# Half transposes over two PSUM banks, and a deeper attention pipeline

## What is computed

```
# attention: 2 batches, 8 heads, 768 positions, 64 channels, fp32
keep = (key < n_global=8) | (0 <= query - key < n_local=96)
scores = q @ k.T / 8 - slope[head] * dist;  a = softmax over the kept keys
x = (a @ v), heads side by side                   # 1536 tokens x 512
# feed-forward 1: a rational function as activation
h = x @ w_in                                      # 1536 x 2048
g = (a0 + a1 h + a2 h^2 + a3 h^3) / (1 + |b0||h| + |b1| h^2 + 1e-6)
y = g @ w_out                                     # 1536 x 512
# feed-forward 2
h = y @ w2_in; s = h * softmax(h); ln = layernorm(s) * g_ln; out = ln @ w2_out
```

## Time and profile before

| | before |
|---|---|
| median of 3 runs | 491.24 us |
| profiled execution, its own time | 491.82 us |
| its span | 489.9 us |
| PE busy | 480.8 us (98%) |
| DVE busy | 380.6 us (78%) |
| ACT busy | 262.9 us (54%) |
| POOL busy | 63.0 us (13%) |

### The profile page before, as it was taken

How to read it: one execution, slowest core, us unless ns; L and a number is a source line. 1 busy time by engine, 2 the same in 40 slices (tenths; PEclk the granted TensorE clock), 3 DMA queues, 4 the chain that set the end, 5 groups by cost and what they waited for, 6 DMA issues and landing times.

```text
span 489.9 us, 7177 instructions
## 1 busy us (share of the span) xinstructions
PE 480.8 (98%) x2560; PEld 390.8 (80%) x2560; DVE 380.6 (78%) x705; ACT 262.9 (54%) x474; POOL 63.0 (13%) x133
## 2 busy tenths in 40 slices
PE   7999999999999999999999999999999999999997
PEld 5777667888888887888888788888888888888885
DVE  5899996899999789888878999999785554554450
ACT  4999895655454556544545655444444333433341
POOL 4767765200000000000000000000000000000000
PEclk9999999999999999999999999999999999999999
DMA  8699969600000000000032336332012222222201
GB/s 289 212 400 416 406 233 373 223 34 0 1 0 1 1 0 1 0 1 0 1 87 86 113 102 193 88 110 84 0 44 64 66 65 64 64 64 64 73 34 43
DMA packets 26959, 50.22 MB, mean 103 GB/s; under 512 B 2224, under 2 KB 16560, under 8 KB 25392
## 3 DMA queue, kind: packets, MB, share of 16 engines
q1 hardware_dynamic: 23760, 37.23, 21.9%
q0 software_dynamic: 2880, 12.58, 7.6%
q10 hardware_dynamic: 288, 0.01, 0.0%
HBM read 40.38 MB, written 3.15 MB: 89 GB/s over the span
## 4 chain that ended last, share of the span: by engine, by line
PE 86%; DVE 11%; ACT 2%; issue 1%; POOL 0%; POOLq 0%; DVEq 0%
PE ps L1102 9%; PE ps L1104 9%; PE ps L1103 9%; PE ps L1032 8%; PE ps L1033 8%; PE ps L1034 8%; PE ps L1167 4%; PE ps L1165 4%; PE ps L1122 4%; PE ps L1166 4%; PE ps L1121 4%; PE ps L1120 4%; DVE negs L653 3%; PE ps L1148 2%; DVE bank_a_lo L690 2%; PE ps L963 2%
## 5 line engine op out<-in xcount | busy, mean ns | idle before, releaser
L1102 PE MATMUL ps<-gate_hi,bank_b_hi 128*128 128x512 f32 x192 | 74.8, 390 | 0.5 <-DVE tok_lo L852 0.5
L1032 PE MATMUL ps<-tok_hi,bank_a_hi 128*128 128x512 f32 x192 | 75.1, 391 | 0.0
L1033 PE MATMUL ps<-tok_lo,bank_a_hi 128*128 128x512 f32 x192 | 74.7, 389 | 0.0
L1034 PE MATMUL ps<-tok_hi,bank_a_lo 128*128 128x512 f32 x192 | 74.7, 389 | 0.0
L1103 PE MATMUL ps<-gate_lo,bank_b_hi 128*128 128x512 f32 x192 | 74.7, 389 | 0.0
L1104 PE MATMUL ps<-gate_hi,bank_b_lo 128*128 128x512 f32 x192 | 74.7, 389 | 0.0
L494 ACT ACTIVATE quad<-ps 128x1024 f32<-128x1024 f32 x24 | 24.7, 1029 | 69.9 <-DVE rest L794 67.0
L412 POOL TENSOR_SCALAR probs<-probs,small 128x256 f32<-128x256 f32 (+1 forms) x96 | 48.6, 519 | 24.7 <-DVE small L663 24.0
L452 ACT ACTIVATE probs<-negs,small 128x256 f32<-128x256 f32 (+1 forms) x96 | 46.1, 485 | 6.0 <-DVE small L653 5.7
L776 DVE SCALAR_TENSOR_TENSOR quad<-quad,small,absh 128x1024 f32<-128x1024 f32 x24 | 30.8, 1283 | 21.5 <-ACT absh L497 21.4
L497 ACT ACTIVATE absh<-ps,small 128x1024 f32<-128x1024 f32 x24 | 26.8, 1116 | 33.8 <-PE ps L1104 33.8
(11 more groups left out here) (94 smaller groups left out, 948.3 us busy)
## 6 DMA issues: line engine op xcount, KB each, us to landing
v_sb<-in_v_win SPq DMA_DIRECT2D x8, 704.0 KB, 7.6
bank_a_raw<-in_w_in SPq DMA_DIRECT2D x4, 1024.0 KB, 11.2
bank_a_hi<-in_w_in POOLq DMA_DIRECT2D x4, 1024.0 KB, 9.9
bank_b_raw<-in_w_out SPq DMA_DIRECT2D x4, 1024.0 KB, 9.8
bank_b_hi<-in_w_out POOLq DMA_DIRECT2D x8, 512.0 KB, 5.6
q_sb<-in_q_t SPq DMA_DIRECT2D x16, 192.0 KB, 5.9
k_sb<-in_k_win SPq DMA_DIRECT2D x8, 384.0 KB, 7.2
stage_hi<-tok_hi SPq DMA_DIRECT2D x12, 256.0 KB, 2.7
```

Source lines behind the costliest of these rows:

```text
L1032: pe.matmul(banks(bank, 1), bank_a_hi[:, f, ws], x_hi, start=(k == 0), stop=False)
L1033: pe.matmul(banks(bank, 1), bank_a_hi[:, f, ws], x_lo, start=False, stop=False)
L1034: mm = pe.matmul(banks(bank, 1), bank_a_lo[:, f, ws], x_hi, start=False, stop=(k == KT - 1))
L1102: pe.matmul(banks(4 + k, 1), bank_b_hi[:, f, ws], g_hi, start=first, stop=False)
```

## The change

Each 128x128 transpose becomes two half transposes: rows 0 to 63 (queries) into bank 4 and rows 64 to 127 into bank 5, with 64 moving columns each. A pair of blocks fills both banks, and then ACT copies all of bank 4 and DVE all of bank 5 (for each pair one copy of 128x512 on either engine; 384 wide where the first block of six is in the pair). The banks no longer alternate by block: the transposes of a pair wait for both copies of the pair before. Sums and reciprocals are made once for a pair. Scores run eight blocks ahead instead of six and exponentials six instead of four, with 8 probability buffers; the transposed tiles move to the upper half of `bank_b_raw`'s place, so the second half of w_out is loaded only after the attention. Nine of the 16 low parts of the first weight go to POOL, one behind the normalizing of every fourth block from block 11 on, and the other seven to DVE in iterations 42, 44 and 46 (2, 2 and 3). The casting transfers are issued at blocks 4, 16, 28 and 34. `up(1)` moves behind the values of 46 and 47. The raw w_in transfers keep their place in SP's order.

```diff
--- before.py
+++ after.py
@@ -84,13 +84,12 @@
...
-    PB, TB = 5, 4
+    PB, TB = 8, 4
...
-    spare = iter(range(w, WORK + 22 * KB, SLICE))
-    probs = [at(f"probs{i}", [P, 2, WIN], F32, next(spare)) for i in range(PB - 1)]
-    probs_t = {i: at(f"probs_t{i}", [P, 2 * WIN], F32, next(spare)) for i in (2, 3, 0, 1)}
-    probs += [at(f"probs{PB - 1}", [P, 2, WIN], F32, next(spare))]
+    probs = [at(f"probs{i}", [P, 2, WIN], F32, w + i * SLICE) for i in range(PB)]
+    w += PB * SLICE
+    probs_t = [at(f"probs_t{i}", [P, 2, 2 * WIN], F32, B_LO + 16 * KB + i * 2 * SLICE) for i in range(TB)]
@@ -173,6 +172,10 @@
...
+    def turned_at(n, r, first):
+        return banks(4 + r, 1)[:, n % 2 * WIN + first * D:n % 2 * WIN + (first + 1) * D]
@@ -226,16 +230,22 @@
...
-    AHEAD, SCORES_AHEAD, SUMS_AHEAD = 4, 6, 2
...
-    SPLIT_FROM, CAST_FROM, CAST_EVERY = 16, 10, 6
+    POOL_IN, SPLIT_FROM, SPLIT_EVERY = 9, 11, 4
+    CASTS_AT = (4, 16, 28, 34)
+    LATE_IN = ((POOL_IN, POOL_IN + 2), (POOL_IN + 2, POOL_IN + 4), (POOL_IN + 4, FT))
+    def outs_at(n):
+        return [m for m in range(2, DONE_B0 - 1, 3) if n == m + (3 if m % 2 else 4)] + \
+            [m for m in (DONE_B0 - 1,) if n == HEADS - 4]
@@ -282,13 +292,15 @@
...
-            load_w_out()
+            load_w_out(0, 2)
+            sp.wait_ge(values_ready, HEADS)
+            load_w_out(2, 4)
@@ -398,6 +410,12 @@
...
+        def split_in_low(f):
+            pool.wait_ge(in_loaded[f // 4], 16)
+            pool.wait_ge(in_hi_loaded[f // 4], 16)
+            pool.tensor_tensor(bank_a_lo[:, f, :], bank_a_raw[:, f, :], bank_a_hi[:, f, :].bitcast(F32),
+                               ALU.subtract).then_inc(in_lo_pool, 1)
@@ -406,19 +424,23 @@
...
-                pool.wait_ge(dve_step, n * STEPS_PER_BLOCK + SETUP_STEPS + 2)
...
-                    pv = probs[pbuf][:, h, lo:WIN]
-                    pool.tensor_scalar(pv, pv, prec[pbuf][:, h:h + 1], 1.0, ALU.mult, ALU.mult).then_inc(probs_ready, 1)
-                i, part = divmod(n - CAST_FROM, CAST_EVERY)
-                if part == 0 and 0 <= i < 4:
-                    cast_w_in(i)
+                    pv, j = probs[pbuf][:, h, lo:WIN], n % 2 * 2 + h
+                    pool.tensor_scalar(pv, pv, prec[n // 2 % (PB // 2)][:, j:j + 1], 1.0, ALU.mult, ALU.mult).then_inc(probs_ready, 1)
+                if n in CASTS_AT:
+                    cast_w_in(CASTS_AT.index(n))
+                f, part = divmod(n - SPLIT_FROM, SPLIT_EVERY)
+                if part == 0 and 0 <= f < POOL_IN:
+                    split_in_low(f)
@@ -449,18 +471,16 @@
...
         def attend_copy(n):
-            if n % COPY_EVERY == COPY_EVERY - 1:
-                return
-            act.wait_ge(turned_ready, n + 1)
-            src, dst = banks(4 + n % 2, 1), probs_t[n % TB][:]
-            if n % BLOCKS == 0:
-                src = src.rearrange("p (h c) -> p h c", h=2)[:, :, P:WIN]
-                dst = dst.rearrange("p (h c) -> p h c", h=2)[:, :, P:WIN]
+            lo = 0 if n % BLOCKS else P
+            act.wait_ge(turned_ready, n + 2)
+            src = banks(4, 1)[:, lo:2 * WIN].rearrange("p (c q) -> p c q", q=D)
+            dst = probs_t[n // 2 % TB][:].rearrange("p u (c q) -> p (u c) q", q=P)[:, lo // D:, 0:D]
@@ -471,18 +491,18 @@
...
-        def attend_unit(n):
+        def attend_pair(n):
             k = n + AHEAD
+            for m in outs_at(n):
+                attend_out(m)
             if k < HEADS:
-                attend_exp(k, 0)
-            if n % 3 == 0 and 6 <= n < HEADS - 3:
-                attend_out(n - 4)
-            elif n == HEADS - AHEAD:
-                attend_out(DONE_B0 - 1)
+                for h in range(2):
+                    attend_exp(k, h)
             attend_copy(n)
             if k < HEADS:
-                attend_exp(k, 1)
+                for h in range(2):
+                    attend_exp(k + 1, h)
@@ -648,6 +668,8 @@
...
+            if h == 0 and n >= 2:
+                dve.wait_ge(exp_ready, 2 * (n - 1))
@@ -655,22 +677,19 @@
...
         def attend_sums(n):
-            dve.wait_ge(exp_ready, 2 * n + 2)
-            dve.tensor_scalar(psums_eps[n % PB], psums[n % PB], 1e-9, None, ALU.add).then_inc(dve_step, 1)
+            dve.wait_ge(exp_ready, 2 * n + 4)
...
         def attend_copy(n):
-            if n % COPY_EVERY != COPY_EVERY - 1:
-                return
-            dve.wait_ge(turned_ready, n + 1)
-            src, dst = banks(4 + n % 2, 1), probs_t[n % TB][:]
-            if n % BLOCKS == 0:
-                src = src.rearrange("p (h c) -> p h c", h=2)[:, :, P:WIN]
-                dst = dst.rearrange("p (h c) -> p h c", h=2)[:, :, P:WIN]
+            lo = 0 if n % BLOCKS else P
+            dve.wait_ge(turned_ready, n + 2)
+            src = banks(5, 1)[:, lo:2 * WIN].rearrange("p (c q) -> p c q", q=D)
+            dst = probs_t[n // 2 % TB][:].rearrange("p u (c q) -> p (u c) q", q=P)[:, lo // D:, D:P]
@@ -709,16 +727,19 @@
...
-                if m in (BLOCKS + 2, BLOCKS + 3) and pr + 1 < PAIRS:
-                    attend_bias(pr + 1, m - (BLOCKS + 2), OF_FIRST)
-            if n % 3 == 1 and 7 <= n < HEADS - 3:
-                attend_low(n - 5)
-            elif n == HEADS - AHEAD:
-                attend_low(DONE_B0 - 1)
+                    dve.wait_ge(bias_ready, 4 * pr + 4)
             attend_copy(n)
-            f, part = divmod(n - SPLIT_FROM, 2)
-            if part == 0 and 0 <= f < FT:
-                split_in_low(f)
+            if k < HEADS:
+                for h in range(2):
+                    attend_shift(k + 1, h)
+            if k < HEADS and m == BLOCKS + 2 and pr + 1 < PAIRS:
+                for h in range(2):
+                    attend_bias(pr + 1, h, OF_FIRST)
+            for m_out in outs_at(n):
+                attend_low(m_out)
+            if n >= HEADS - AHEAD:
+                for f in range(*LATE_IN[(n - HEADS + AHEAD) // 2]):
+                    split_in_low(f)
@@ -965,23 +988,21 @@
...
         def wait_copied(n):
-            by_dve = (n + 1) // COPY_EVERY
-            if n % COPY_EVERY == COPY_EVERY - 1:
-                pe.wait_ge(turned_copied_dve, by_dve)
-            else:
-                pe.wait_ge(turned_copied_act, n + 1 - by_dve)
+            pe.wait_ge(turned_copied_act, n // 2 + 1)
+            pe.wait_ge(turned_copied_dve, n // 2 + 1)
...
         def attend_turn(n):
...
-            if n >= 2:
+            if n >= 2 and n % 2 == 0:
                 wait_copied(n - 2)
             for h in range(2):
                 pe.wait_ge(probs_ready, 2 * n + h + 1)
                 for half in range(0 if i else 1, 2):
-                    c = h * WIN + half * P
-                    mm = pe.transpose(banks(4 + n % 2, 1)[:, c:c + P], probs[n % PB][:, h, half * P:(half + 1) * P],
-                                      ident[:])
+                    for r in range(2):
+                        rows = slice(r * D, (r + 1) * D)
+                        mm = pe.transpose(turned_at(n, r, 2 * half + h), probs[n % PB][rows, h, half * P:(half + 1) * P],
+                                          ident[rows, rows])
...
         def attend_values(n):
@@ -997,8 +1018,8 @@
...
-                    c = h * WIN + half * P
-                    mm = pe.matmul(dst, v_sb[b][:, v_block, h * D:(h + 1) * D], probs_t[n % TB][:, c:c + P],
+                    c = (2 * half + h) * P
+                    mm = pe.matmul(dst, v_sb[b][:, v_block, h * D:(h + 1) * D], probs_t[n // 2 % TB][:, n % 2, c:c + P],
@@ -1045,11 +1069,10 @@
...
-                if n == HEADS - 2:
-                    pe.wait_ge(shifted_ready, 2 * HEADS)
-                    up(1)
             for n in (HEADS - 2, HEADS - 1):
                 attend_values(n)
+            pe.wait_ge(shifted_ready, 2 * HEADS)
+            up(1)
```

70 lines of the change are left out of this document (40 added, 30 removed).

## The result

The changed kernel takes 498.29 us, the median of four runs (497.00 to 499.48), against 491.09 us (490.91 to 491.75) for the kernel before on the same chip: ratio 1.0144, with an interval of 1.0117 to 1.0171. It is slower, and 10.2 us above the predicted 488.1. The profiled execution took 498.22 us, its span 496.4 us, 6.5 us more than before.

A forecast was written before the change was run, and what follows sets the result against it. PE, ACT and DVE were nearly full; ACT would set the pace afterwards. `up(0)` 3.1 us earlier, transposes 0.4 shorter, a 0.35 wait: net 3.15 off 491.82 gives 488.7 profiled, 488.1 median; range 485.0 to 492.0, own range 486.7 to 490.0.

The forecast's parts named there:

- the pace of 2.68 us an iteration: Attention iterations after the change: ACT's 2.59 us plus 0.09 for ACT and DVE taking turns, over 14 iterations.
- the clock: PE's clock, granted in full before the change; the sum adds no time for a fall to half rate.
- the stretch before `up(0)`: From the copy of pair 40 to `up(0)`: 5.4 us, with DVE the longest, so `up(0)` starts at 75.9.
- The wait on POOL: POOL's first subtraction, behind block 11, waits for w_in's first quarter, landing at 29.7 to 31.1: 3.0 us lost once.
- The rival with chance 0.10: Before iteration 12 PE idles, the clock falls to 1.2 GHz for one iteration, costing about 2.5 us: 490.6; chance 0.10.
- if ACT and DVE hold each other up by more than 0.2 us an iteration: In the attention's iterations: a listed sign that the prediction is wrong, more than 0.2 us an iteration.
- ACT's own sum: ACT in the attention: exponentials, copies and outputs of six blocks take 7.77 us, 2.59 an iteration, setting the pace.
- DVE's 7.3 us for six blocks: DVE in the attention: fewer weight parts and sums, longer copies, giving 7.3 us for six blocks, 2.45 an iteration.
- POOL's subtraction: On POOL in the attention: one two-input subtraction of 512 columns takes 1.2 us, bounds 0.65 to 1.3.
- The half transposes: On PE in the attention: transposes of a full pair take 0.6 us instead of 1.02, half tiles running side by side.
- The wait at `up(4)`: Behind `up(1)`: `up(4)` waits 0.35 us for the first gate's poly, done 5.8 us after `up(1)`.
- the transposes behind `up(0)`: Behind `up(0)`: the transposes of blocks 46 and 47 are 0.4 us shorter.

The follow-up runs named there:

- kernel 1: Changed kernel with the first quarter of the raw w_in issued before all of SP's waits: 492.89 us, ratio 1.0015.
- kernel 6: Changed kernel with the early first w_in quarter, no epsilon addition, and all seven of DVE's low parts in iteration 46: 486.73 us, ratio 0.9898.
- kernels 6 and 9: The former is kernel 6; the latter is the changed kernel with only DVE's seven low parts moved to iteration 46: 496.63 us, ratio 1.0099.
- kernel 4: Changed kernel with eighteen extra matmuls, results unread, keeping PE busy before iteration 12: 497.93 us, ratio 1.0124.
- kernel 10: Kernel 6 with only four of POOL's nine low parts in the attention and five behind its last normalizing: 488.86 us, ratio 0.9941.
- kernel 11: Kernel 10 with four of DVE's seven low parts at the end of iteration 44, three in 46: 486.09 us, ratio 0.9909.
- kernel 2: Changed kernel without POOL's nine subtractions, PE reading the high part in their place: 487.39 us, ratio 0.9921.
- kernel 5: Changed kernel with the first w_in quarter issued early and the epsilon addition left out: 488.37 us, ratio 0.9936.
- see 7: Kernel 5 with whole 128x128 transposes again, block n into bank 4 and n+1 into bank 5: 491.56 us, ratio 1.0002.
- kernel 3: Changed kernel without the addition of epsilon (1e-9) to the softmax sums: 495.94 us, ratio 1.0084.
- kernel 12: Kernel 6 with four of DVE's seven low parts at the end of iteration 44: 486.77 us, ratio 0.9908.

## Why the prediction was wrong

Two steps of the sum failed most: the pace of 2.68 us an iteration, which let POOL's subtractions cost DVE nothing, and the clock, which the sum left at full speed throughout. A third, the stretch before `up(0)`, failed by less. By its own steps, against the profiled execution (488.7 predicted, 498.22 measured, 9.5 more):

- **The wait on POOL: right.** Landing at 30.2 (29.7 to 31.1 forecast) and the subtraction ending at 31.5 (30.9). Against kernel 1 iteration 12 is 3.15 us late, 3.0 forecast.
- **The clock: put at nothing in the sum, and held too unlikely.** The rival with chance 0.10 came in full: iteration 12 took 5.29 us, 2.6 more than the forecast pace, and iteration 14 still 0.4 more than the twelve behind it. A second fall, at `up(0)`, was in no case of mine. Nine of its matmuls take 0.43 us instead of 0.23: 1.8 us. The traces show what PE did before: 4.48 us idle the first time; the second time, short waits one after another from 75 to 83 us (of the transposes 0.38, 0.71 and 1.08, then 0.54), with transposes of 64 columns between them. Where moving DVE's low parts takes that second fall away, the kernel gets 1.6 and 1.7 us faster (kernels 6 and 9); without the first, kernel 4 is no faster.
- **The pace: failed.** "I take 2.68 us an iteration" had DVE's epsilon operation at its own length whatever POOL does. It was 2.94, 13 x 0.26 = 3.4 us more. The text named the sign of it, "if ACT and DVE hold each other up by more than 0.2 us an iteration", but not its cause. ACT's own sum was sound: with no subtraction beside it and no epsilon, kernels 10 and 11 run at 2.59 us an iteration, which is ACT's figure to the second place, and kernel 2 at 2.73. DVE's 7.3 us for six blocks was not what its terms add up to (8.9 - 2.34 - 0.27 + 0.75 = 7.04, 2.35 an iteration instead of 2.45), which changed nothing in a sum that went by ACT.
- **The stretch before `up(0)`: too short.** From the copy of pair 40 to `up(0)` I had 5.4 us, all of it DVE's work. It took 7.25 (76.36, DVE's copy, to 83.61), 1.85 more, and the chain is POOL's. POOL's end of the attention, DVE's first two low parts, and the eight last normalizings in kernel 6:

```profile
77.80 1.28 POOL L416 TENSOR_TENSOR bank_a_lo<-bank_a_raw,bank_a_hi 128x512 fp32r<-128x512 f32 x1
79.05 4.64 POOL L430 TENSOR_SCALAR probs<-probs,small 128x256 f32<-128x256 f32 x8
```

```profile
79.87 1.28 DVE L708 TENSOR_TENSOR bank_a_lo<-bank_a_raw,bank_a_hi 128x512 fp32r<-128x512 f32 x2
```

```profile
70.13 3.65 POOL L431 TENSOR_SCALAR probs<-probs,small 128x256 f32<-128x256 f32 x8
```

  POOL has no pause from 77.80 to 83.69. Its third normalizing takes 1.46 us instead of 0.48 beside DVE's two low parts: the same hold, the other way round. Without DVE's low parts there the eight take 3.65 us and the stretch 6.28 (kernel 6); without POOL's subtraction too, 5.48 (kernel 10), the forecast's 5.4.
- **POOL's subtraction: right** at 1.28 us for 1.2.
- **The half transposes: right.** A full pair takes 0.64 us to the values behind it (0.6 forecast). Their loads last 138 ns, as long as those of whole transposes (140) and longer than the 107 that the prediction cites, but they overlap, sixteen of them in 0.64 us, so they don't set the pace. They are worth 3.2 us in kernel 5 (see 7).
- **The wait at `up(4)`: right,** 0.45 for 0.35; the transposes behind `up(0)` too (0.64 instead of 1.02).

The terms add up. The copies of pair 12, ACT's and DVE's, start at 33.70, 0.7 later than forecast; from there to DVE's copy of pair 40 are 42.66 us instead of 37.5, 5.1 more, of which the pace is 3.4 (0.4 of it the half clock of iteration 14) and iteration 12 the other 1.7; the last stretch 1.85, the half clock at `up(0)` 1.8, the wait 0.1. That is 9.55, and 9.5 were missing. This is a sum over one trace. Taken away one at a time they are not independent: the clock's 2.4 us of iterations 12 and 14 were gone by iteration 36 in kernel 4, and kernel 3 has a shorter pace but the same stall.

**The cause of the pace.** What the runs show is this. An operation of DVE that reads and writes SBUF only, of the kinds tensor_scalar (L681, L661) and tensor_tensor (L707), waits for POOL's subtraction to end if it begins inside it; the one at 66.40 waited for the rest of POOL's normalizing as well. The reciprocal (0.17 us) and the operations that read PSUM (the shift at 0.41, the copy at 0.69) don't. In the other direction POOL's normalizing had a mean of 572 ns from 34 to 79 us before, while DVE made low parts beside it, and 488 in the changed kernel. Moving nine two-input operations from DVE to POOL therefore takes 0.78 us each off DVE and puts time back on it whenever one of those small operations comes due meanwhile: 0.7, 0.9, 0.9, 1.0 and 1.6 us in the five cases of the changed kernel.

The Trainium skill states the rule: in "SBUF — State Buffer" (SBUF: two separate sides) the port pair that DVE and GpSimd share is an exclusive lock, held for a whole instruction, against DVE operations in a two-port mode or, where GpSimd's operation reads SBUF, with two SBUF inputs, and "the other fully blocks". A two-port mode is one that fp32 tensor_scalar from SBUF to SBUF enters ("VectorE: DVE Perf Modes", Mode 2x_2P), and a source in PSUM excludes it. This case agrees: 1.82 us for an operation of 0.2, 7.75 us instead of 4.29, and none of it on operations that read PSUM. Why the reciprocal escapes, no run here shows. It also agrees on what gets through, since in kernel 11 the two engines' own times fill the stretch from 72.89 to 81.96 (9.07 us): POOL's 6.38, and of DVE's 4.53 (2.65 + 1.88 in kernel 12) the 2.5 that were left at 72.89. I had cited only the length of POOL's operation. With the lock in the sum, the forecast would have held an epsilon operation in every second iteration for up to 1.28 us behind POOL, up to 0.64 us an iteration on a DVE at 2.35 to 2.45, which is 3.0 to 3.1: the case of no gain. It came to less, because four of the nine subtractions caught no such operation.

**Open.** What makes the clock fall at `up(0)` in some kernels and not in others. Why the edits of 1 and 3 give more together than alone. And what the 0.14 us an iteration are by which kernel 2 stays above ACT's 2.59: its epsilon operations, or transfers of k that it ran into sooner.
